# Splitting two weight matrices in place for the first batch of a fused attention and MLP kernel

## The reference

```
# attention: q, k, v are (4, 8, 576, 64)
phi(x) = concat(exp(p), exp(-p)),  p = x @ w_phi - max|x @ w_phi|
kv = phi(k)^T v ;  z = sum over tokens of phi(k)
x  = (phi(q) kv) / (phi(q) z + 1e-6)               -> (4, 576, 512)
# MLP 1: w_in (512, 1024), conv_w (3, 1024), w_out (1024, 512)
h  = relu(x @ w_in)
x1 = (h * sigmoid(conv over 3 tokens of h)) @ w_out
# MLP 2: U (576, 32), V (32, 576), w_ch1 (512, 2048), w_ch2 (2048, 512)
u  = x1 + ((x1^T U) V)^T
out = u + relu(u @ w_ch1) @ w_ch2
```

## Time and profile before

| | us |
|---|---|
| median of 3 runs | 872.88 |
| lowest and highest run | 869.78, 873.67 |
| the profiled execution, on the device | 871.45 |
| its span | 869.8 |
| TensorE busy in it | 842.3 (97%) |
| VectorE, ScalarE, GpSimd busy | 373.1, 290.4, 101.3 |

### The profile page before, as it was taken

How to read it: one execution, slowest core, us unless ns; L and a number is a source line. 1 busy time by engine, 2 the same in 40 slices (tenths; PEclk the granted TensorE clock), 3 DMA queues, 4 the chain that set the end, 5 groups by cost and what they waited for, 6 DMA issues and landing times.

```text
span 869.8 us, 17287 instructions
## 1 busy us (share of the span) xinstructions
PE 842.3 (97%) x7394; PEld 820.4 (94%) x7394; DVE 373.1 (43%) x641; ACT 290.4 (33%) x581; POOL 101.3 (12%) x67
## 2 busy tenths in 40 slices
PE   7987999999999999999999999999999999999997
PEld 6876999989999899999999999999999999999997
DVE  6673585466854658546954432212212112122111
ACT  3563464345643456435523321111111111111111
POOL 5443121001210012100410010100100010010000
PEclk9998999999999999999999999999999999999999
DMA  8999632338223481145745401101101101201001
GB/s 189 271 261 231 202 98 79 87 102 275 69 79 87 113 269 37 55 165 165 253 145 175 133 3 61 49 1 55 56 1 49 61 1 37 73 1 37 37 1 36
DMA packets 106043, 89.10 MB, mean 102 GB/s; under 512 B 61041, under 2 KB 92657, under 8 KB 103921
## 3 DMA queue, kind: packets, MB, share of 16 engines
q1 hardware_dynamic: 105216, 87.82, 33.8%
q10 hardware_dynamic: 752, 0.20, 0.1%
HBM read 70.18 MB, written 17.83 MB: 101 GB/s over the span
## 4 chain that ended last, share of the span: by engine, by line
PE 82%; DVE 10%; issue 3%; ACT 3%; DMA 0%; SPq 0%; POOL 0%; ACTq 0%; DVEq 0%
PE qnb L1061 8%; PE qnb L1059 8%; PE qnb L1060 8%; PE pjb L1059 6%; PE pjb L1061 5%; PE mb L1059 5%; PE pjb L1060 5%; PE mb L1061 5%; PE mb L1060 5%; PE qnb L1066 4%; PE kvb L1066 4%; DVE cv L868 2%; PE tpb L1059 2%; PE kvb L1061 2%; PE tpb L1061 2%
## 5 line engine op out<-in xcount | busy, mean ns | idle before, releaser
L980 DVE SCALAR_TENSOR_TENSOR c_lo<-qnb,c_hi 128x384 fp32r<-128x384 f32 x94 | 52.4, 558 | 282.7 <-ACT c_hi L757 282.7
L757 ACT ACTIVATE c_hi<-qnb 128x384 fp32r<-128x384 f32 x94 | 46.3, 492 | 294.2 <-PE qnb L1061 290.3
L1059 PE MATMUL qnb<-u_hi,w_b 128*128 128x384 f32 x384 | 129.7, 338 | 0.0
L1061 PE MATMUL qnb<-u_hi,w_b 128*128 128x384 f32 x384 | 128.4, 334 | 0.0
L1060 PE MATMUL qnb<-u_lo,w_b 128*128 128x384 f32 x384 | 128.4, 334 | 0.0
L526 POOL TENSOR_TENSOR g_lo<-cv,g_hi 128x576 fp32r<-128x576 f32 x31 | 46.2, 1491 | 315.8 <-DVE g_hi L799 315.8
L1059 PE MATMUL mb<-x_hi,winr 128*128 128x288 f32 x224 | 69.6, 311 | 5.1 <-DMA winr<-wi_dram 5.1
L1060 PEld LDWEIGHTS qnb<-u_lo,w_b 128*128 128x128 f32 x384 | 72.1, 188 | 0.0
L1059 PEld LDWEIGHTS qnb<-u_hi,w_b 128*128 128x128 f32 x384 | 72.1, 188 | 0.0
L1061 PEld LDWEIGHTS qnb<-u_hi,w_b 128*128 128x128 f32 x384 | 72.1, 188 | 0.0
L814 DVE TENSOR_REDUCE nm<-pjb 128x4 f32<-128x512 f32 (+1 forms) x80 | 50.6, 632 | 46.9 <-PE pjb L1061 46.4
(11 more groups left out here) (256 smaller groups left out, 1896.7 us busy)
## 6 DMA issues: line engine op xcount, KB each, us to landing
winr<-wi_dram SPq DMA_DIRECT2D x32, 512.0 KB, 4.4
woutr<-wo_dram SPq DMA_DIRECT2D x15, 1024.0 KB, 6.2
stage<-in_moe_w_ch_dram SPq DMA_DIRECT2D x32, 256.0 KB, 3.8
us<-u_dram SPq DMA_DIRECT2D x6, 768.0 KB, 4.7
ua<-u_dram SPq DMA_DIRECT2D x6, 768.0 KB, 4.7
qr<-in_q_dram SPq DMA_DIRECT2D x32, 128.0 KB, 2.7
vt<-in_v_dram SPq DMA_DIRECT2D x32, 128.0 KB, 3.3
wi_dram<-aw SPq DMA_DIRECT2D x8, 512.0 KB, 5.5
```

What stands on the lines that cost most here:

```text
L757: nc.scalar.activation(c_hi[:, j % CR, :], CH[j % 2][:, 0:TW], ACT.Relu).then_inc(s_chh, 1)
L980: nc.vector.scalar_tensor_tensor(out=c_lo[:, j % CR, :], in0=CH[j % 2][:, 0:TW], scalar=0.0, in1=c_hi[:, j % CR, :].bitcast(F32), op0=ALU. ...
L1059: mm(o, a_hi, b_hi, start=start, stop=False)
L1061: return mm(o, a_lo, b_hi, start=False, stop=stop)
```

## The change

`astage`, `aw`, `fetch`, `put_back` and `prepare` go. For batch 0, SyncE loads a raw tile (`raw_in` 256 KB, `raw_out` 512 KB, in runs of 512 bytes) into one of three places (rooms of x1 that are free until the first `outputs` has ended, and a room of its own) or into the one place for `w_out`. GpSimd splits it straight into its slot of `winr` or `woutr`, where batch 0's product reads it (`split_in`, `split_out`). SyncE stores the slot from there as one DMA (`put_in`, `put_out`) for the batches that follow. Tiles 0 to 2 of `w_in` and 0 and 1 of `w_out` are split ahead of GpSimd's gates, tile n+3 ahead of `gate_low(n)` for n from 0 to 4, and tiles 2 and 3 of `w_out` behind `gate_low(7)`. GpSimd prepares U and V first, and the constants are loaded behind group 1's loads. A piece of hidden channels is now 128 neighbours rather than every eighth, so `conv_w` is loaded element by element. The first transposes of x1's second group go from (16, 0) to (15, 2).

```diff
-    def put_tick(n):
-        return 4 + 2 * n
+    RAW_IN = {5: 0, 6: 1, 7: 2, 12: 3, 14: 4, 16: 5, MLP0 + 2: 6, MLP0 + 3: 7}
+    RAW_OUT = {9: 0, 18: 1, 22: 2, MLP0 + 12: 3}
+    PUT_IN = {MLP0 - 3 + j if j < WR else MLP0 + j - 1: j for j in range(J1)}
+    PUT_OUT = {MLP0 + 2: 0, MLP0 + 4: 1, MLP0 + 13: 2, MLP0 + 15: 3}
...
     X1_AT = {(12, 0): (0, 0), (12, 1): (0, 1), (13, 1): (0, 2),
-             (16, 0): (1, 0), (16, 1): (1, 1), (17, 0): (1, 2)}
+             (15, 2): (1, 0), (16, 1): (1, 1), (17, 0): (1, 2)}
...
+        wout_raw = raw[:, 0:J1 * P]
+        win_raw = [x1[:, 2, 0:C], x1[:, 3, 0:C], raw[:, J1 * P:J1 * P + C]]
...
+            def raw_in(j):
+                sp.wait_ge(s_wil, max(0, j - WR + 1))
+                sp.dma_start(win_raw[j % WR].rearrange("p (c m) -> p c m", m=P),
+                             w_in[:, j * P:(j + 1) * P].rearrange("(c p) m -> p c m", p=P)
+                             ).then_inc(s_wir[j % WR], 16)
+
+            def raw_out(c):
+                sp.wait_ge(s_wol, c)
+                sp.dma_start(wout_raw.rearrange("p (j m) -> p j m", m=P),
+                             w_out[:, c * P:(c + 1) * P].rearrange("(j p) m -> p j m", p=P)).then_inc(s_wor, 16)
+
+            def put_in(j):
+                sp.wait_ge(s_wil, j + 1)
+                sp.dma_start(wi_dram[:, j, :, :, :], winr[:, j % WR, :, :, :].bitcast(F32)).then_inc(s_wist[j % WR], 16)
+
+            def put_out(c):
+                sp.wait_ge(s_wol, c + 1)
+                sp.dma_start(wo_dram[:, c, :, :, :], woutr[:, c % 2, :, :, :].bitcast(F32)).then_inc(s_wost[c % 2], 16)
...
-            sp.dma_start(cw[:, :, :], conv_w.rearrange("k (p j) -> p k j", j=J1)).then_inc(s_const_ld, 16)
+            sp.dma_start(cw[:, :, :], conv_w.rearrange("k (j p) -> p k j", p=P),
+                         allow_slow_non_contiguous=True).then_inc(s_const_ld, 16)
...
             def weights(tick):
-                if tick == MLP0 - 3:
-                    load_win(0, 0)
-                    load_win(0, 1)
-                if 0 <= b < B - 1:
-                    if m < J1 and b + m // 2:
+                if tick in PUT_IN:
+                    put_in(PUT_IN[tick])
+                if tick in PUT_OUT:
+                    put_out(PUT_OUT[tick])
+                if tick in RAW_IN:
+                    raw_in(RAW_IN[tick])
+                if tick in RAW_OUT:
+                    raw_out(RAW_OUT[tick])
+                if 0 < b < B - 1:
+                    if m < J1:
                         load_win(b, m)
...
+            def split_in(j):
+                hi, lo = [winr[:, j % WR, s, :, :].rearrange("p c m -> p (c m)") for s in range(2)]
+                pool.wait_ge(s_wir[j % WR], 16 * (j // WR + 1))
+                if j >= WR:
+                    pool.wait_ge(s_hid, 2 * (j - WR + 1))
+                    pool.wait_ge(s_wist[j % WR], 16 * (j // WR))
+                nc.gpsimd.tensor_copy(hi, win_raw[j % WR]).then_inc(s_wih, 1)
+                pool.wait_ge(s_wih, j + 1)
+                sub(lo, win_raw[j % WR], hi.bitcast(F32)).then_inc(s_wil, 1)
+
+            def split_out(c):
+                hi, lo = [woutr[:, c % 2, s, :, :].rearrange("p j m -> p (j m)") for s in range(2)]
+                pool.wait_ge(s_wor, 16 * (c + 1))
+                if c >= 2:
+                    pool.wait_ge(s_oc, 2 * (c - 1))
+                    pool.wait_ge(s_wost[c % 2], 16)
+                nc.gpsimd.tensor_copy(hi, wout_raw).then_inc(s_woh, 1)
+                pool.wait_ge(s_woh, c + 1)
+                sub(lo, wout_raw, hi.bitcast(F32)).then_inc(s_wol, 1)
...
+            for j in range(WR):
+                split_in(j)
+            for c in range(2):
+                split_out(c)
             for n in range(J1 * B - 1):
+                if n + WR < J1:
+                    split_in(n + WR)
                 gate_low(n)
+                if n == J1 - 1:
+                    split_out(2)
+                    split_out(3)
...
                 if half + quarters.start == 0:
-                    pe.wait_ge(s_wi[n % WR], winr_loads(b, j))
+                    if b:
+                        pe.wait_ge(s_wi[n % WR], winr_loads(b, j))
+                    else:
+                        pe.wait_ge(s_wil, j + 1)
```

More of the change, by code:

```diff
@@ L157, in winr_loads @@
     def winr_loads(b, j):
-        return 16 * ((J1 * b + j) // WR + 1)
+        return 16 * ((J1 * (b - 1) + j) // WR + 1)
     def woutr_loads(b, c):
-        return 16 * ((CC * b + c) // 2 + 1)
-    def stored(n):
-        return 16 * sum(2 if m < CC else 4 for m in range(n % 2, n, 2))
+        return 16 * ((CC * (b - 1) + c) // 2 + 1)
     ctx = ExitStack()
@@ L202, in program @@
         rden = sb("rden", [P, 2, TM + 1], F32, ph_a)
-        sb("a_room", [P, 7 * 2 * P], F32, ph_a)
+        raw = sb("a_room", [P, 7 * 2 * P], F32, ph_a)
         winr = sb("winr", [P, WR, 2, CC, P], F32R, ph_a)
@@ L290, in program @@
         s_fill, s_ident, s_zero, s_phi = sem("fill"), sem("ident"), sem("zero"), sem("phi")
-        s_ast, s_awh, s_awl = [sem(f"ast{n}") for n in range(SLOTS)], sem("awh"), sem("awl")
-        s_wst = [sem("wst0"), sem("wst1")]
+        s_wir, s_wih, s_wil = [sem(f"wir{n}") for n in range(WR)], sem("wih"), sem("wil")
+        s_wor, s_woh, s_wol = sem("wor"), sem("woh"), sem("wol")
+        s_wist, s_wost = [sem(f"wist{n}") for n in range(WR)], [sem("wost0"), sem("wost1")]
         s_wl = sem("wl")
@@ L346, in load_v @@
                              ).then_inc(s_vld[g % 2], 16)
[L348 to L370, removed]
@@ L372, in load_win @@
+            def put_in(j):
[4 more added lines that the diff above has]
+                sp.dma_start(wo_dram[:, c, :, :, :], woutr[:, c % 2, :, :, :].bitcast(F32)).then_inc(s_wost[c % 2], 16)
             def load_win(b, j):
                 n = J1 * b + j
-                if n < WR:
-                    sp.wait_ge(s_wst[0], stored(NA))
-                    sp.wait_ge(s_wst[1], stored(NA + 1))
+                if (b, j) == (1, 0):
+                    for i in range(WR):
+                        sp.wait_ge(s_wist[i], 16 * len(range(i, J1, WR)))
@@ L381, in load_wout @@
                 n = CC * b + c
+                if (b, c) == (1, 0):
+                    for i in range(2):
+                        sp.wait_ge(s_wost[i], 16 * len(range(i, CC, 2)))
                 sp.wait_ge(s_oc, max(0, 2 * (n - 1)))
@@ L407, in _ @@
             load_v(1)
+            sp.dma_start(u_raw[:, 0:UT - 1, :],
+                         U[0:(UT - 1) * P, :].rearrange("(t p) r -> p t r", p=P)).then_inc(s_const_ld, 16)
+            sp.dma_start(u_raw[token_tile(UT - 1)[1], UT - 1, :],
+                         U[(UT - 1) * P:S, :]).then_inc(s_const_ld, 16)
+            for n in range(4):
+                sp.dma_start(v_raw[n * R:(n + 1) * R, :], V).then_inc(s_const_ld, 16)
+            sp.dma_start(cw[:, :, :], conv_w.rearrange("k (j p) -> p k j", p=P),
+                         allow_slow_non_contiguous=True).then_inc(s_const_ld, 16)
             def weights(tick):
                 b, m = divmod(tick + 2 - MLP0, BATCH)
-                if tick == MLP0 - 3:
-                    load_win(0, 0)
-                    load_win(0, 1)
-                if 0 <= b < B - 1:
-                    if m < J1 and b + m // 2:
+                if tick in PUT_IN:
[8 more added lines that the diff above has]
+                    if m < J1:
                         load_win(b, m)
@@ L442, in _ @@
                     load_v(g + 2)
-                for n in range(NA):
-                    if tick == put_tick(n):
-                        put_back(n)
                 weights(tick)
```

25 lines of the change are left out of this document (3 added, 22 removed).

## The result

The changed kernel takes 857.16 us, the median of 4 runs (856.26 to 858.08), against 873.27 us for the kernel before on the same chip (4 runs, 869.78 to 873.94): a ratio of 0.983, interval 0.981 to 0.985. The forecast was 861.0 us. The kernel before and the changed one are compared by medians of their runs, or between profiles; a single profiled execution can lie 1 to 2 us from another of the same kernel.

The account below looks back on a forecast made before the run. TensorE was taken as the bound, with SyncE's queue behind its gap near 62 us. 12.84 + 1.4 - 3.1 = 11.1 us off 871.45 gives 860.3, from the 872.88 median 861.7; forecast 861.0 us, range 856 to 867.5.

Parts of the forecast that it names:

- The two stalls at the front: Up to batch 0's first product: waits at kvb and for winr go, with the clock loss behind, 12.84 us gained.
- Rival (c): The gap at 62 us is not SyncE's doing and stays, DMA engines full; 5.2 us more, 866 us; chance 0.08.
- The splits: GpSimd's splits beside the convolution's taps in batch 0 delay VectorE, and through it TensorE: 3.1 us lost.
- my turns: Tap, cast, tap, subtraction alternate; the pair ends 0.4, 1.5, 0.9 and 1.3 us later beside tiles 4 to 7.
- x1's second group: Earlier first transposes in batches 0 and 1 remove a 1.42 us wait, half given back: 1.4 us gained in all.
- Priced at nothing: conv_w's 4-byte packets ahead of group 2's keys, and the last w_out piece with 2.9 us spare: 0 us.
- rival (d): Slower: conv_w's 4-byte packets delay group 2's loads; at 150 ns a packet 18 us late, 879 us; chance 0.06.
- rival (a): GpSimd's splits in batch 0 cost nothing: about 858 us; chance 0.2.

Follow-up runs that it names:

- e8: The kernel before with w_out stores in 4 issues and an eighth of the bytes: span 858.4 us against 869.8.
- e6: The kernel before with all bytes of the w_out stores in 4 issues of 1 MB: span 864.5 us against 869.8.
- e5: The kernel before with all 16 w_out store issues but a quarter of the bytes: span 866.2 us against 869.8.
- e2: The kernel before with only x1's second group's first transposes moved to (15, 2): 869.38 us, ratio 0.998.
- e3: The changed kernel with tiles 4 to 7 of w_in split in only 16 of 512 columns: 854.77 us, ratio 0.982 to the kernel before.
- e9: The changed kernel with tiles 3 to 7 split in the attention phase, second raw w_out piece earlier: 854.77 and 854.23 us.
- e1: The changed kernel with x1's second group's first transposes put back to (16, 0): 858.48 us, ratio 0.986 to the kernel before.
- e4: The changed kernel with the subtraction of tiles 4 to 7 done twice: 859.71 us, span 857.9.
- e7: The changed kernel with conv_w loaded four times, three of them into an unread buffer: 859.86 us, span 858.1.

## Why the prediction was right, and where it was not

**The two stalls at the front.** The size held: 12.84 us forecast, 13.09 us measured, all three parts whole (13.07 us for the group, no wait for winr, 6.20 us between the first tiles). The 0.25 us more lies between group 5's transposes and the first product: 9.77 us before, 4.68 without the wait of 5.09, and 4.42 now.

The cause as I put it, "SyncE's queue is the bound there, one instruction of it behind another", holds as far as it goes: the value tile of group 4 was issued 16.4 us later than now, and with the w_out stores thinned out in both ways (e8) the gap and the wait for winr are gone. It is not the whole. I read the lateness from one row, four stores in 4.61 us, but the queue was already 9.1 us behind the new one at the tile of group 3. And I counted issues only: fewer issues alone (e6) leave 3.54 of 4.08 us of the gap, fewer bytes alone (e5) 1.25 of 2.83. The change took away both. I had also written that "full DMA engines as such do not slow a group", from a group of 13.07 us at 1.02. That group had its tiles ahead of need; the next no longer had. Rival (c) was wrong in its result, since the gap went, but right that the bytes have a part in it. The gains don't add up: e6 saves 5.3 us of span against the kernel before; against e2 with x1's 2.2 us put back (871.2 us) e5 saves 5.0 us and e8 12.8.

**The splits.** 3.1 us forecast, 1.98 measured. The place and the kind were right: one tap of 1.80 us in place of 0.81, pairs of taps of 2.60 and 2.57 us and one of 1.95, a wait for x_lo in tick 31, and with the splits nearly gone (e3) or elsewhere (e9) it all goes. The term was too high in how much of VectorE's delay reaches TensorE. I took 2.8 us of lateness to show whole at x_lo, and 0.98 us did (1.44 - 0.46), with 0.23 us more for dq and 0.1 for xl_lo; the rest of the 1.98 us lies in no wait long enough to be listed. VectorE's own loss was 3.3 us, where my turns made 4.1 (0.4, 1.5, 0.9 and 1.3 for tiles 4 to 7): by the timelines of the changed kernel and of e3 the taps lose 1.0, 0.9, 0.2 and 0.9, and the gate beside tile 6 0.3. Twice the subtraction costs 1.72 us more, so the cost goes on rising with GpSimd's time; but it comes from the gate and from g_hi, no longer from the taps.

The Trainium skill says in "SBUF — State Buffer", section "Who interferes with whom", that a VectorE instruction with two SBUF inputs and a GpSimd one that reads SBUF exclude each other. This trace agrees: 1.66 us for a pair alone, 2.60 us beside a subtraction that took 1.68 in place of 1.28 us. Each pays for the other, in turns.

**x1's second group.** 1.4 us forecast, 2.2 measured, by e1 and e2 in both directions. I let half of the 1.42 us come back at xl_lo. The wait there is 0.17 us in the changed kernel, so 1.25 of 1.42 us should stay, and 1.1 us a batch did. The low half and the add delayed VectorE by less than the 1.9 us I added.

**Priced at nothing.** conv_w cost nothing that shows: one load takes about 2.2 us of the queue, out of the 14 us between the issue of group 2's keys (15.88 us) and their use (29.96 us). Three more cost 3.7 us of span. My 17 to 26 ns a packet was too high for 4 bytes, and rival (d) is further off than I had it. The last w_out piece was ready at 150.9 us, 4.2 us ahead of its use at 155.11, where I had allowed 2.9: its raw load landed in 4.2 us, not 5.5.

**Not in the prediction: the constants behind group 1.** I noted that they move and gave it no price. In the profiled pair it has none, since both had the late clock. In the others it is worth more: with the early clock the kernel before gains nothing and is even 1.6 to 1.9 us later at group 4, and the changed kernel gains 1.9 us. That fits the differences between the medians, 16.1, 13.7 and 14.5 us in the three comparisons, being above the 13.5 us of the pair, though the second hardly is. It rests on profiles; a kernel with this part alone was not run, and why the clock of one start comes late stays open.

**The sum.** 13.09 - 1.98 + 2.22 = 13.3 us, with 0.2 us elsewhere, against 11.1 us forecast: 1.1 us too dear for the splits, 0.8 and 0.25 too little for x1 and the front; and up to 2.6 us of the medians is the start's. The 857.16 us lie nearer to the 858 us of rival (a) than to my 861.0, but not for its reason: the splits cost 2.0 us, and the misses of splits, x1, front and start happen to point the same way.

## What to carry to other kernels

When a queue looks late, ask two things of it, how many issues stand ahead and how many bytes they move: here taking away one left a good part of the stall, taking away both left none, and the parts' gains did not add. Look also at when the queue began to fall behind, not only at the issue ahead of the stall. Put GpSimd's elementwise work where VectorE has no instruction with two SBUF inputs, nor a cast from SBUF to SBUF (e4); moving five splits by some ticks was worth 2.0 us of 856. Profile a kernel more than once before pricing its first microseconds: a start that varies by 1.9 us can hide, or feed, a wait of the old kernel.

## What the runs showed of the hardware that I had not expected

- The issue of one DMA on SyncE can take three times as long, and the share of the DMA engines alone does not say when: 0.61 us for a store of 128 KB in e8, 1.96 us for one of 1 MB in e6 in the same place, both with the DMA engines full; two key loads take 1.28 us before, at a share of 0.45 (18 to 20 us), and 3.56 us behind conv_w's 3072 packets.
- A packet of 4 bytes costs 10.3 ns of a DMA engine, under the 17 ns of packets of about 250 bytes, but nearly 40 times as much for each byte: a load of 12 KB holds the queue for 2.2 us (e7).
- GpSimd pays as VectorE does: a cast of 0.61 us took 1.20 beside a tap, a subtraction of 1.28 took 1.80. A VectorE cast from SBUF to SBUF with one input was held as well, 1.43 us in place of 0.46 beside GpSimd's subtraction (e4).
- The same program reached its steady pace 1.9 us sooner or later; 1.5 us of it went with the granted clock after 11 us, 0.50 or 1.00 behind the same 1.9 us of idle TensorE. In e4 the clock stayed at 1.00 behind 2.38 us.
